# Attention and two expert layers on one core: output products spread over the common tile, the first head begun in pieces, one copy moved up

## The reference

```python
def _attn_ref(q, k, v):
    B, H, S, D = q.shape                        # 2, 8, 1152, 64
    q_pool = q.reshape(B, H, S // 2, 2, D).mean(axis=3)
    scores = (1.0 / np.sqrt(D)) * np.matmul(q_pool, k.transpose(0, 1, 3, 2))
    scores = scores - np.max(scores, axis=-1, keepdims=True)
    attn = np.exp(scores)
    attn = attn / (np.sum(attn, axis=-1, keepdims=True) + 1e-09)
    return np.matmul(attn, v)

def _moe_ref(x, w_gate, w_val, w_out):          # 1152 x 512, 512 x 1536 twice, 1536 x 512
    gate = 1.0 / (1.0 + np.exp(-(x @ w_gate)))
    return gate * (x @ w_val) @ w_out

def _moe2_ref(x, w_gate, w1, w2):               # 8 experts, 512 x 1024 and 1024 x 512
    P = np.exp(x @ w_gate - (x @ w_gate).max())
    for _ in range(8):
        P /= P.sum(1, keepdims=True) + 1e-09
        P /= P.sum(0, keepdims=True) + 1e-09
        P *= N / E
    for e in range(E):
        out += P[:, e:e + 1] * (np.maximum(x @ w1[e], 0.0) @ w2[e])
```

## Time and profile before

| | |
|---|---|
| median of 3 runs | 1274.16 us (1273.3 to 1277.93) |
| the profiled execution | 1273.37 us, its span 1271.5 us |
| attention (first score to the last) | 11.1 to about 282 us of the span |
| gated layer | to about 508 us |
| experts | to the end |
| busy PE, DVE, ACT, POOL | 98%, 60%, 46%, 45% of the span |

### The profile page before, as it was taken

One profiled execution on the slowest core, in us unless ns is written; L12 is line 12 of the kernel. 1 busy time (PEld: TensorE's weight loads), 2 busy tenths in 40 slices (PEclk: granted clock), 3 DMA queues, 4 the chain that ended last, 5 costly groups with the idle time before them and its releaser, 6 DMA issues.

```text
span 1271.5 us, 19547 instructions
## 1 busy us (share of the span) xinstructions
PE 1243.0 (98%) x7492; PEld 1137.6 (89%) x7492; DVE 761.5 (60%) x1642; ACT 584.9 (46%) x1232; POOL 571.3 (45%) x340
## 2 busy tenths in 40 slices
PE   6999999999999999999999999999999999999998
PEld 5888888889999989998998999999999999999997
DVE  5999999982222332767566565475465466466443
ACT  5999899863333224543344233234234234233221
POOL 2678778841212256544335245245146245245220
PEclk9999999999999999999999999999999999999999
DMA  6788887312110232123122122122122122122112
GB/s 159 119 107 111 102 114 105 71 37 83 34 49 16 84 99 76 50 67 84 51 74 76 51 84 67 50 84 67 51 83 67 50 84 76 43 82 83 49 35 92
DMA packets 97175, 94.24 MB, mean 74 GB/s; under 512 B 14272, under 2 KB 71616, under 8 KB 97088
## 3 DMA queue, kind: packets, MB, share of 16 engines
q1 hardware_dynamic: 96928, 92.48, 31.3%
q10 hardware_dynamic: 160, 0.59, 0.2%
HBM read 88.59 MB, written 2.40 MB: 72 GB/s over the span
## 4 chain that ended last, share of the span: by engine, by line
PE 84%; DVE 12%; ACT 3%; DMA 1%; issue 0%; ACTq 0%
PE bank L938 11%; PE bank L940 11%; PE bank L939 11%; PE bank L1092 10%; PE bank L1093 10%; PE bank L1094 10%; DVE part_min L1424 5%; PE bank L915 4%; PE bank L916 4%; PE bank L917 4%; DVE pT_lo L1375 3%; PE bank L840 3%; PE bank L827 2%; PE bank L841 2%; PE bank L806 2%; ACT probs L1170 2%
## 5 line engine op out<-in xcount | busy, mean ns | idle before, releaser
L1541 DVE TENSOR_TENSOR c<-bank,c 128x256 f32<-128x256 f32 (+1 forms) x448 | 197.4, 457 | 284.2 <-PE bank L940 275.2
L765 POOL TENSOR_TENSOR w_lo<-w_raw,w_hi 128x1024 fp32r<-128x1024 f32 x64 | 153.9, 2405 | 300.7 <-ACT w_hi L1109 300.7
L1092 PE MATMUL bank<-w_hi,h_hi 128*128 128x512 f32 x576 | 224.9, 390 | 0.0
L1093 PE MATMUL bank<-w_lo,h_hi 128*128 128x512 f32 x576 | 224.8, 390 | 0.0
L1094 PE MATMUL bank<-w_hi,h_lo 128*128 128x512 f32 x576 | 224.1, 389 | 0.0
L1285 ACT ACTIVATE h_hi<-c 128x256 fp32r<-128x256 f32 (+1 forms) x256 | 112.7, 445 | 166.4 <-DVE c L1541 166.1
L1094 PEld LDWEIGHTS bank<-w_hi,h_lo 128*128 128x128 f32 x576 | 108.2, 188 | 23.0
L1092 PEld LDWEIGHTS bank<-w_hi,h_hi 128*128 128x128 f32 x576 | 108.4, 188 | 20.8
L1093 PEld LDWEIGHTS bank<-w_lo,h_hi 128*128 128x128 f32 x576 | 108.4, 188 | 20.1
L1424 DVE TENSOR_REDUCE part_min<-bank 128x1 f32<-128x256 f32 (+2 forms) x216 | 113.1, 555 | 19.5 <-PE bank L841 16.5
L1109 ACT ACTIVATE c<-bank 128x256 f32<-128x256 f32 (+1 forms) x64 | 26.2, 410 | 209.8 <-PE bank L940 209.8
(11 more groups left out here) (145 smaller groups left out, 3024.0 us busy)
## 6 DMA issues: line engine op xcount, KB each, us to landing
w_raw<-in_moe_w SPq DMA_DIRECT2D x64, 512.0 KB, 3.6
w_raw<-in_moe_w SPq DMA_DIRECT2D x64, 256.0 KB, 3.2
q_raw<-in_q SPq DMA_DIRECT2D x32, 288.0 KB
k_raw<-in_k SPq DMA_DIRECT2D x30, 288.0 KB, 8.8
wo_raw<-in_moe_w_out SPq DMA_DIRECT2D x16, 384.0 KB, 3.4
v_raw<-in_v SPq DMA_DIRECT2D x16, 288.0 KB, 8.8
gv_raw<-in_moe_w_gate SPq DMA_DIRECT2D x12, 256.0 KB, 2.9
gv_raw<-in_moe_w_val SPq DMA_DIRECT2D x12, 256.0 KB, 3.2
```

The source lines that it names most:

```text
L765: nc.gpsimd.tensor_tensor(w2_lo[:, u % 2], w2_raw[:], f32(w2_hi[:, u % 2]), ALU.subtract).then_inc(w2_split, 1)
L1092: nc.tensor.matmul(bank[:, 3 + i], hh, wh, start=first, stop=False)
L1093: nc.tensor.matmul(bank[:, 3 + i], hh, wl, start=False, stop=False)
L1541: nc.vector.tensor_tensor(dst[:, 0:w], bank[:, (u + b) % 3, 0:w], other[:, 0:w], ALU.add).then_inc(done, 1)
```

## The change

Three parts. First, the number of output steps in each slot becomes a list: (9, 9, 9, 9, 6, 6, 6, 9, 9), and (9, 9, 9, 9, 9, 9, 0, 9, 9) in the last pair, so the common tile's slot gets 6 (9), and the waits ahead of the steps are split so that the last piece of the low parts is waited for only at the steps that read it. Second, head 0's q and k come in two pieces each, on semaphores of their own: 256 columns of q, which do for the first two tiles, and 640 keys; the rest of q is summed by GpSimd, and its high and low parts are made in the first and second tile. SP now loads q of head 1 ahead of k of head 1. TensorE runs 26 transposes ahead of the first scores in place of 16, and 9 in each of slots 0 to 3 of the first pair. Third, `p1_copy(1)` stands ahead of `w1_hi_sums(3)`.

```diff
-AV_STEPS = 9
+AV_STEPS = (9, 9, 9, 9, 6, 6, 6, 9, 9)
+AV_STEPS_LAST = (9, 9, 9, 9, 9, 9, 0, 9, 9)
+WARM_UP, WARM_TILE = 26, 9
+Q_BEGIN = 2 * PARTS
...
             def load_kq(h):
+                if h == 2:
+                    sp.wait_ge(q_begin_summed, 1)
                 sp.wait_ge(q_summed[h > 2], max(h - 2, 1))
...
-            load_q(0)
+            for cols, done in ((slice(0, Q_BEGIN), q_begin_loaded), (slice(Q_BEGIN, QLEN), q_loaded[0])):
+                for half in range(2):
+                    sp.dma_start(q_raw[0][rows_of(half), :, cols], q_dram[0][:, :, cols]).then_inc(done, 16)
+            load_q(1)
             load_k(1)
-            load_q(1)
             load_v(0)
...
+            rest = slice(Q_BEGIN, QLEN)
+            pool.wait_ge(q_loaded[0], 32)
+            nc.gpsimd.tensor_tensor(q_sum[0][:, rest], q_raw[0][:, 0, rest], q_raw[0][:, 1, rest],
+                                    ALU.add).then_inc(q_summed[0], 1)
             sum_q(1)
...
-                    pe.wait_ge(p_lo_done, 3 * (PAIR * (h // 2) + AV_TILES[a][u]))
+                    own_bank = h == NHEAD - 1 and u == 0
+                    pe.wait_ge(p_lo_done, 3 * (PAIR * (h // 2) + AV_TILES[a][u]) - (0 if own_bank else 1))
...
+                if c == KEYS[2] // PARTS and not lo:
+                    pe.wait_ge(p_lo_done, 3 * (PAIR * (h // 2) + AV_TILES[a][u]))
...
                 if i in (0, COMMON):
-                    pe.wait_ge(q_lo_done, h + 1)
+                    if g == 0:
+                        pe.wait_ge(q_begin_lo_done, 1)
+                    else:
+                        pe.wait_ge(q_lo_done, h + 1)
                     pe.wait_ge(*k_there(h, 1))
+                if g == Q_BEGIN // PARTS:
+                    pe.wait_ge(q_lo_done, 1)
...
+                steps = AV_STEPS_LAST if pair == NHEAD // 2 - 1 else AV_STEPS
                 if i < COMMON and pair >= 1:
-                    for n in range(AV_STEPS * i, AV_STEPS * (i + 1)):
-                        av(h - 1, n)
-                if i > COMMON:
-                    for n in range(AV_STEPS * (i - COMMON - 1), AV_STEPS * (i - COMMON)):
-                        av(h - 1, n)
+                    for n in range(sum(steps[:i]), sum(steps[:i + 1])):
+                        av(2 * pair - 1, n)
+                if i < COMMON and pair == 0:
+                    warm(7, WARM_TILE)
+                if i >= COMMON:
+                    for n in range(sum(steps[COMMON:i]), sum(steps[COMMON:i + 1])):
+                        av(2 * pair, n)
+
+            def warm(b, times):
+                for n in range(times):
+                    nc.tensor.transpose(bank[:, b, 0:PARTS], ones[:], ident[:])
...
-            for n in range(16):
-                nc.tensor.transpose(bank[:, 2, 0:PARTS], ones[:], ident[:])
+            warm(2, WARM_UP)
...
             def between(pair, i):
                 h = 2 * pair
+                if i == 0 and pair == 0:
+                    q_hi_part(0)
...
-            for half in range(2):
-                act.dma_start(k_raw[0][rows_of(half)], k_dram[0]).then_inc(k_loaded[0], 16)
+            for piece, done in enumerate((k_begin_loaded, k_loaded[0])):
+                k0, k1 = KPIECES[piece]
+                for half in range(2):
+                    act.dma_start(k_raw[0][rows_of(half), k0:k1], k_dram[0][:, k0:k1]).then_inc(done, 16)
+            act.wait_ge(q_begin_summed, 1)
+            q_scaled(0, slice(0, Q_BEGIN)).then_inc(q_begin_hi_done, 1)
             k_hi_part(0, 0)
-            q_hi_part(0)
             k_hi_part(0, 1)
...
-            w1_hi_sums(3)
             for u in range(1, NUNIT):
                 e, n, m = unit(u)
                 p1_copy(u)
+                if u == 1:
+                    w1_hi_sums(3)
                 w2_hi_part(u)
...
+                if g == 1:
+                    q_lo_part(0)
                 if i in (1, 6) and h < NHEAD - 1:
                     q_lo_part(h + 1)
...
-            dve.wait_ge(q_loaded[0], 32)
-            nc.vector.tensor_tensor(q_sum[0][:], q_raw[0][:, 0], q_raw[0][:, 1], ALU.add).then_inc(q_summed[0], 1)
-            for piece in range(2):
-                st, raw = k_of(0, piece)
-                dve.wait_ge(k_hi_done, piece + 1)
-                lo_part(st[rows_of(0)], raw[rows_of(0)], st[rows_of(0)], k_lo_done[0])
-                if piece == 0:
-                    q_lo_part(0)
+            dve.wait_ge(q_begin_loaded, 32)
+            first = slice(0, Q_BEGIN)
+            nc.vector.tensor_tensor(q_sum[0][:, first], q_raw[0][:, 0, first], q_raw[0][:, 1, first],
+                                    ALU.add).then_inc(q_begin_summed, 1)
+            dve.wait_ge(q_begin_hi_done, 1)
+            q_part(0, first).then_inc(q_begin_lo_done, 1)
+            split_first_k(0)
+            split_first_k(1)
```

More of the change, by code:

```diff
@@ L234, in build @@
         q_loaded = [sem(f"q_loaded{a}") for a in range(2)]
+        k_begin_loaded = sem("k_begin_loaded")
+        q_begin_loaded = sem("q_begin_loaded")
+        q_begin_summed = sem("q_begin_summed")
+        q_begin_hi_done = sem("q_begin_hi_done")
+        q_begin_lo_done = sem("q_begin_lo_done")
         v_loaded = sem("v_loaded")
@@ L1114, in q_hi_part, with q_scaled @@
                 act.wait_ge(q_summed[h > 0], max(h, 1))
-                nc.scalar.activation(q_hi[h % 2][:, q_cols(h % 2)], q_sum[h % 2][:], ACT.Copy,
-                                     scale=-SCALE).then_inc(q_hi_done, 1)
+                cols = slice(0 if h else Q_BEGIN, QLEN)
+                q_scaled(h, cols).then_inc(q_hi_done, 1)
+            def q_scaled(h, cols):
+                at = slice(q_cols(h % 2).start + cols.start, q_cols(h % 2).start + cols.stop)
+                return nc.scalar.activation(q_hi[h % 2][:, at], q_sum[h % 2][:, cols], ACT.Copy, scale=-SCALE)
             def k_hi_part(h, piece):
-                act.wait_ge(k_loaded[h % 2], 32 * (h // 2) + 32)
+                if h == 0 and piece == 0:
+                    act.wait_ge(k_begin_loaded, 32)
+                else:
+                    act.wait_ge(k_loaded[h % 2], 32 * (h // 2) + 32)
                 copy(*k_of(h, piece)).then_inc(k_hi_done, 1)
@@ L1377, in q_lo_part, with q_part, split_first_k @@
             def q_lo_part(h):
+                dve.wait_ge(q_hi_done, h + 1)
+                q_part(h, slice(0 if h else Q_BEGIN, QLEN)).then_inc(q_lo_done, 1)
+            def q_part(h, cols):
                 a = h % 2
-                dve.wait_ge(q_hi_done, h + 1)
-                nc.vector.scalar_tensor_tensor(q_lo[a][:, q_cols(a)], q_sum[a][:], -SCALE, f32(q_hi[a][:, q_cols(a)]),
-                                               ALU.mult, ALU.subtract).then_inc(q_lo_done, 1)
+                at = slice(q_cols(a).start + cols.start, q_cols(a).start + cols.stop)
+                return nc.vector.scalar_tensor_tensor(q_lo[a][:, at], q_sum[a][:, cols], -SCALE, f32(q_hi[a][:, at]),
+                                                      ALU.mult, ALU.subtract)
+            def split_first_k(piece):
+                st, raw = k_of(0, piece)
+                dve.wait_ge(k_hi_done, piece + 1)
+                lo_part(st[rows_of(0)], raw[rows_of(0)], st[rows_of(0)], k_lo_done[0])
             def p_lo(g, j):
```

## The result

The changed kernel takes 1268.78 us (median of 11 runs), the kernel before 1274.18 (median of 11, the three above among them). The ratio is 0.9956, with a 95% interval of 0.9943 to 0.9969. The forecast was 1269.2 in a range of 1265.8 to 1274.0, with "within 0.5%" as the likeliest case. One of the 11 runs, 1352.1 us, was taken in a disturbed state and is left out of every comparison. The profiled execution took 1269.04 us, its span 1267.2: 4.33 us less than the profiled one before.

What follows compares the result with a forecast made beforehand. TensorE was taken to bound the kernel from 545 us, VectorE most of each attention pair. Terms 2.15 + 1.9 + 0 + 0.4 = 4.45 us took the profiled 1273.37 to 1268.9; median forecast 1269.2, range 1265.8 to 1274.0.

Steps and rivals of the forecast that it cites:

- within 0.5%: Whole kernel: time changes by no more than 0.5%, 6.4 us, either way; chance 0.73.
- Part 1, 0: Output steps in slot 4 of the attention: gain 0, as VectorE sets tiles 5 to 8.
- The transfers: Start: q's first pieces complete at 5.4 us, all eight at 8.8; `nmax` of tile 0 at 12.0, gain 2.15.
- The clock, 1.9: Tiles 1 to 3: full clock from 13 to 15 us, intervals 10.4 in all; gain 2.3, 1.9 counted, at most 2.7.
- The second rival: First tiles: clock stays low as long as before, the start's gain is gone, 1273.0 us; chance 0.17.
- the third: Attention: clock low beyond tile 2, slower, 1279.9 us through tile 4; chance 0.04.
- part 2: The start: gains of 2.15 us from loading in pieces and 1.9 us from the clock.
- Part 3, 0.4: Experts, P1 copied first: 2.6 us vanish in unit 1, waits return in units 2 and 3; gain 0.4.
- The allowance for held-up low parts: Attention, 11 to 282 us: GpSimd holds up a few low-part instructions by about 1 us; number can change by two.

Runs made afterwards that it cites:

- e7b_act_and_tb: Changed kernel with ScalarE's unit 2 copy and unit 3 exponential reordered, and GpSimd's TB_lo behind unit 3's w2 low parts: 1269.82 us, ratio 0.9959.
- e4_act_order: Changed kernel with P1's unit 2 copy ahead of TB_hi and the logits' exponential behind the unit 3 copy on ScalarE: 1269.08 us, ratio 0.9948.
- e2_p1_only: Kernel before with only the copy of P1 of unit 1 moved ahead of the sums' high part: 1275.01 us, ratio 0.9994.
- e1_av_back: Changed kernel with the output steps put back, none in slot 4 and nine in slots 5 to 8, last pair too: 1271.12 us, ratio 0.9958.
- e3_no_tile_standins: Changed kernel without the nine stand-in transposes in slots 0 to 3 of the first pair, the 26 at the start kept: 1271.9 us, ratio 0.9969.

## Why the prediction was right

By its steps:

- **Part 1, 0.** Right. The shortest intervals of tiles 5 to 8 are 3.31, 3.31, 3.65 and 3.28 us after and stay so with the steps put back; VectorE's tiles set them, as the earlier trace rows said. The last pair, for which 0.1 to 0.3 us of loss were allowed, lost nothing: its tiles 4 to 8 take what they took before. One sign did not come: TensorE was to idle more in slots 5 and 6. The wait of 0.92 us ahead of tile 5's scores is gone and no other of its size has come; over tiles 5 to 8 of an undisturbed pair TensorE is idle for 0.42 us where it was 0.98. Busy says only that matmuls were in flight, so this row can't settle which engine sets the tiles; the unchanged intervals do.

```profile
188.09:201.65 13.56, 13.14 (x91) 11.12 (x88) 13.14 (x31) 12.99 (x33) 12.16 (x9) 1.00 0.75 89
```

- **The transfers.** q's first pieces were used at 6.45 us, 1.0 us later than the 5.4 of the prediction; k's second piece at 8.11, 0.7 earlier than 8.8. The trace's landings tell the order: k's two first pieces were complete at 5.45 us, q's at 6.35, k's second at 8.09, and all eight pieces at 8.75, as predicted (8.8). The total was right; the order of landing in equal steps of 1.3 us, read from two transfers, did not carry over to the pieces. First scores 8.95 in place of 8.0, `nmax` of tile 0 11.84 in place of 12.0: the step that counts, k's second piece, was off by 0.16 us. Gain 2.31 (2.13 with the pieces alone, at 12.02), predicted 2.15.
- **The clock, 1.9.** That the clock would rise early and leave VectorE's intervals was right; when, and so the size, was not: the term is 2.7, the upper bound. The rise was put into tile 1, at 13 to 15 us, by the only row that showed one, in a stretch of scores and transposes. It came at 5.68 us, within the transposes, and again at 12.50. With the clock high from slot 1 on, all three intervals are VectorE's. The transposes, faster for it, ended at 6.86 and not at 8.0; the 2.10 us without work that followed were followed by a low clock until 12.50. In `e7b_act_and_tb`, where 2.26 us were not, `nmax` of tile 0 came at 11.38, with first scores at 8.71 in place of 8.95: the low stretch cost some 0.2 us from the first scores to `nmax` (2.89 in place of 2.67), and 0.5 in `e4_act_order` (3.16).
- **The rule of the Trainium skill**, "TensorE: Matmul & The Clock Gate", section "PE-mode transpose", that the full clock does not engage for transposes: this case shows the opposite. With nothing but transposes done, the clock rose at 4.86 us (stand-ins alone) and at 5.68 us (the changed kernel). In all seven executions with 26 or 40 transposes it rose ahead of the first scores. The 16 transposes of the earlier trace rows left it low in all three executions that have them; they ended at 5.71 us, and in four of the seven the rise came later than that. That they merely ended too early is the likely reading, not a shown one. The second rival, built on those 16, has fallen with it, and with it the third.
- **The two gains of part 2 are not a sum of two causes.** The pieces alone gave 2.13 + 1.40 us to `nmax` of tile 3, the stand-ins alone 2.61 (26.86 to 24.25), both together 4.98 (26.86 to 21.88). Of what the clock gives back, 2.7 us, the pieces alone already had 1.4.
- **Part 3, 0.4.** Right: 0.55 and, alone, 0.56. The wait in unit 2 was 1.37 us, as said (1.4). For unit 3 the text spoke of about 2 us, and of 1 us or more among its signs; it was 0.57, and it is the two waits together, 1.94, that make the 2. The cause was right as well: the copy of unit 3 stands behind the largest logit, and this behind three `h_lo` that took 6.27 us here, while GpSimd worked on `TB_lo` for 6.24; with that moved, the wait moved (`e4_act_order`, `e7b_act_and_tb`).
- **The allowance for held-up low parts.** The prediction let them change by about 1 us and two instructions. The stretch from tile 4 to the last tile took 1.33 us more in the profiled execution, 0.41 of it in pair 0 and 0.91 in pairs 1 to 6, where the excess was 4.9 us before and 5.8 after. Nearly all of it is q's low parts on VectorE: what they took over 0.75 us each adds up to 4.6 us in pairs 1 to 6 before, and to 5.7 after. One alone takes up to 1.95 us, in both:

```profile
242.67 1.95 DVE L1432 SCALAR_TENSOR_TENSOR q_lo<-q_sum,q_hi 128x576 fp32r<-128x576 f32 x1
```

  It is noise of the kernel: `e2_p1_only`, whose attention is that of the kernel before, has an excess of 9.1 us, and `e4_act_order` and `e7b_act_and_tb`, whose attention is that of the changed kernel, have 7.7 and 5.5. No part of the change was shown to make it larger. What decides in one execution whether GpSimd or VectorE comes first was not tried.

That the profiled sum came out at 4.33 us for 4.45 is luck: its errors, +0.16, +0.8, +0.2 and -1.33, nearly cancel. Between medians the gain is 5.4 us, which agrees with the terms without the hold-ups, 2.3 + 2.7 + 0.6 = 5.6; the forecast had made it 5.0.

## What to carry to other kernels

An engine that waits for its first data can be kept at dummy work, and near its first tiles too: here forty transposes at the start and nine in each of four slots are worth 2.8 us of intervals, at 0.19 us on the first tile. Put them near the tiles, where the gaps are short: ten more at the start alone, with a wait behind them, brought nothing in the one execution that tells, and the nine a slot, on top of 26, brought 1.1 us. Count the gain of a removed wait only up to the next instruction that did not wait for the engine you freed: of an estimated 2.6 us in unit 1, 0.55 arrived. And time a thing that two engines of shared access do next to each other over several executions, since one execution's sum of such hold-ups moved by more than one part of the change is worth.

## What the runs showed of the hardware

The clock rises for transposes alone, between 4.86 and 8.11 us in the executions with 26 or 40 of them, where TensorE had begun at 2.04. It also falls behind a single wait: 1.09 us in unit 1 before, 1.75 us in the attention of `e1_av_back`, 2.10 us ahead of the first scores, each followed by about 3.4 us at 1.2 GHz, and 1.98 us at the same place in `e3_no_tile_standins`, followed by 6.8. But it doesn't fall for each: 1.37 us in unit 2 left it high, and so did 2.26 us ahead of the first scores of `e7b_act_and_tb`:

```profile
8.71 0.36 PE L865 MATMUL bank<-k_st,q_hi 128*128 128x256 f32 x1 [2.26 <-DVE k_st L1426]
...
10.46 1.15 PE L907 MATMUL bank<-ident,ones 128*128 128x128 f32 x9
```

So the length of the wait alone does not tell.

Instructions of VectorE and GpSimd that both read two tensors of SBUF hold each other up. Three `h_lo`, 1.08 us together when nothing stands beside them, took 3.51 before, 6.27 after; one `q_lo` of 0.75 us took 1.95; and GpSimd's `x_hi` of 1.42 us took 1.80 at 244.08 beside the `q_lo` above. `pT_lo`, which reads one of its two from a bank, kept its 1.48 us for three beside a busy GpSimd (changed kernel, 68.72 us). That the second of the two waits for the whole of the other's instruction fits both groups of `h_lo`: before, `TB_lo` ended at 542.07 and the three `h_lo` 0.95 us later; after, they ended 0.63 us behind the two `TB_lo`. The Trainium skill, "SBUF — State Buffer", section "Who interferes with whom", calls the pair of ports that they share an exclusive lock; these rows agree.
